# Two gate loads merged, the second gate group's sums moved into the prelude, and constants built between the first tiles, in an attention and mixture-of-experts kernel

## The chip, the cores and the metric

One core of one Trainium2 chip. The metric is the device time of one launch in microseconds; for the kernel before, three runs gave a median of 797.4 us (796.29 to 798.65).

## The reference

Three parts follow one another. The first is a gated recurrence over 768 steps for 4 batches of 8 heads of 40 values; the kernel computes it in chunks of 128 steps.

```python
def _attn_ref(q, k, v, i_gate, f_gate, o_gate):
    ...
    for t in range(S):
        m_new = np.maximum(f_gate[:, :, t] + m, i_gate[:, :, t])
        f_stab = np.exp(f_gate[:, :, t] + m - m_new)
        i_stab = np.exp(i_gate[:, :, t] - m_new)
        m = m_new
        C = f_stab[:, :, None, None] * C + i_stab[:, :, None, None] * np.einsum('bhd,bhe->bhde', vt, kt)
        n = f_stab[:, :, None] * n + i_stab[:, :, None] * kt
        h_tilde = np.einsum('bhde,bhe->bhd', C, qt)
        nq = np.einsum('bhd,bhd->bh', n, qt)[:, :, None]
        denom = np.maximum(np.abs(nq), 1.0)
        o = 1.0 / (1.0 + np.exp(-o_gate[:, :, t]))
        y[:, :, t] = o * h_tilde / denom
```

Its 3072 rows of 320 go to a router with 8 experts of capacity 384 each (assignment in falling order of all logits), through the expert's two layers with a rectifier between them, and then through a second pair of layers, 320 to 2048 to 320, with a leaky rectifier. The output is 3072 x 320.

## The kernel before

The program is written by hand for each engine; the order on an engine is the order of its block in the code, and engines meet by semaphores alone. SyncE (SP) issues nearly all loads. Tiles are counted by chunk `c` (6 of them, 128 steps each) and batch `b` (4): tile (c, b) is T = 4c + b, 24 in all.

**Gates.** The running sums of the forget gate, the running maximum and what follows from them are computed ahead for many chunks at once, with (chunk, batch, head) on the partitions: group 0 holds chunks 0 to 3 (128 partitions), group 1 chunks 4 and 5 (64 partitions). `load_gates` (L408) and L959 load them, one DMA per chunk and gate. On VectorE (DVE), `gate_sums(g)` (L1127) makes the sums, `split_peak(g)` (L1142) three bf16 parts of the peak, `fade_weights(g)` (L1154) a diagonal of carry weights, `copy_gates(g)` (L1159) and `copy_fades` (L1167) bring the turned results out of PSUM. ScalarE (ACT) makes exponentials (`gate_weights`, L961) and places the peak parts (`place_peak`, L968). TensorE (PE) turns them (`turn_gates`, L642) and spreads the fade weights over the heads (`spread_fades`, L650).

**A tile.** On PE, `front` (L664) makes the logarithms of the decays (L675) and the scores k.q (L684) of the next tile; `back` (L699) the product with the carried state (L713, from chunk 1 on), the update of the state (L720), the router's logits of the tile two before (L695) and probabilities times v (L732); `turn_x` (L736) turns the output of the tile before (L742). ACT takes exponentials of the decays (L992). DVE multiplies decays and scores (`make_probs`, L1248), then normalises and gates the output of the tile before (`make_x`, L1264), whose first steps read PSUM and write the state. GpSimd (POOL) weighs v (`vw`, L557), masks the probabilities (L563) and fades the state (L570), in `weigh_values` (L548). The loop is software-pipelined by one tile: `step` (L745 on PE, L1306 on DVE, L1010 on ACT) makes the next tile's front before this tile's back. The first four steps are written out; group 1's gate work is hung into them: before the change the sums follow the output of tile (0,0), the split that of (0,1), the fade weights that of (0,2), and the copies that of (0,3); PE turns group 1 in the step of tile (0,3).

**Constants.** POOL fills `ident`, `sel3`, the zero padding and `half_ones`, then all the constants of the routing and of its search (L513 to L546), and only then starts on the tiles (L592).

After tile 23 come the routing search and eight experts, each expert's matmuls in three passes over high and low parts.

## Time and profile before

| what | value |
|---|---|
| median of 3 runs | 797.4 us (796.29 to 798.65) |
| the profiled execution | 797.02 us |
| its span in the trace | 795.3 us |
| PE busy | 741.7 us, 93% of the span |
| DVE busy | 583.1 us, 73% |
| ACT busy | 323.0 us, 41% |
| POOL busy | 160.7 us, 20% |

The span reaches from the first to the last instruction of the trace; 1.7 us of the execution lie outside it. Busy shares are means over stages: attention takes the first 156 us of the span, the routing search and the first rows of an expert some 45 us, the experts the rest.

### The profile page before, as it was taken

The numbers are of one execution on the slowest core, as the hardware profiler recorded it, in microseconds if no ns is written. First come the engines' busy times: TensorE is split into PE (matmuls) and PEld (weight loads), VectorE is DVE, ScalarE is ACT, GpSimd is POOL, SyncE is SP. The second block draws the span as 40 slices with busy tenths as digits, with TensorE's granted clock in tenths as the row PEclk, the third lists the DMA queues.
The fourth block names the chain that finished last, engine by engine and source line by source line (L and its number), as shares of the span: only waits on it lengthen the run. The fifth ranks groups of instructions, "written<-read, shape, count | busy, mean of one in ns | idle before, by whom it ended". The sixth has DMA issues, their size and how long they took to land.

```text
span 795.3 us, 18189 instructions
## 1 busy us (share of the span) xinstructions
PE 741.7 (93%) x6047; PEld 692.6 (87%) x6047; DVE 583.1 (73%) x1615; ACT 323.0 (41%) x775; POOL 160.7 (20%) x240
## 2 busy tenths in 40 slices
PE   5899999752899999999999999999999999999995
PEld 4799999742789998998999899989988998999994
DVE  5878888858578867886887688678867876883442
ACT  5666777301324513441452236134414532361431
POOL 7367777101000220110022002200110220021001
PEclk9999999955899999999999999999999999999998
DMA  6889886103204100400140041004000500310000
GB/s 148 225 251 241 228 228 167 37 12 109 67 2 147 31 26 1 156 26 19 46 129 25 0 132 43 25 0 146 29 25 22 153 25 0 122 52 26 1 1 25
DMA packets 66706, 62.54 MB, mean 79 GB/s; under 512 B 34928, under 2 KB 57840, under 8 KB 66672
## 3 DMA queue, kind: packets, MB, share of 16 engines
q1 hardware_dynamic: 56880, 48.66, 21.6%
q0 software_dynamic: 2688, 8.65, 3.4%
q10 hardware_dynamic: 7104, 4.79, 1.9%
q8 instruction: 20, 0.33, 0.2%
q14 instruction: 14, 0.11, 0.1%
HBM read 53.43 MB, written 8.65 MB: 78 GB/s over the span
## 4 chain that ended last, share of the span: by engine, by line
PE 85%; DVE 8%; issue 2%; ACT 2%; DMA 1%; ACTq 1%; POOL 0%; DVEq 0%; POOLq 0%
PE bank L844 21%; PE bank L846 18%; PE bank L845 18%; PE bank L862 4%; PE bank L863 4%; PE bank L732 4%; PE bank L695 2%; PE bank L713 2%; PE bank L684 2%; PE bank L887 1%; PE bank L888 1%; PE bank L767 1%; PE bank L776 1%; PE bank L838 1%; ACT decay L992 1%
## 5 line engine op out<-in xcount | busy, mean ns | idle before, releaser
L844 PE MATMUL bank<-wo_hi,h_hi 128*128 128x320 f32 x384 | 120.7, 314 | 0.0
L846 PE MATMUL bank<-wo_hi,h_lo 128*128 128x320 f32 x384 | 118.6, 309 | 0.0
L845 PE MATMUL bank<-wo_lo,h_hi 128*128 128x320 f32 x384 | 118.0, 307 | 0.0
L611 POOL DMA_INDIRECT xe<-x_rows,idx_in x24 | 31.1, 1294 | 402.3 <-DVE idx_in L1442 353.4
L1502 DVE SCALAR_TENSOR_TENSOR g_act<-g_neg,rest_alpha,bank 128x384 f32<-128x384 f32 x128 | 78.6, 614 | 39.3 <-ACT g_neg L1075 37.7
L1075 ACT ACTIVATE g_neg<-bank 128x384 f32<-128x384 f32 x128 | 62.8, 491 | 102.1 <-PE bank L863 102.1
L1073 ACT ACTIVATE h_hi<-bank 128x384 fp32r<-128x384 f32 x64 | 31.5, 492 | 163.4 <-PE bank L863 163.4
L1079 ACT CAST h_hi<-g_act 128x384 fp32r<-128x384 f32 x128 | 65.5, 512 | 78.8 <-DVE g_act L1502 78.3
L844 PE MATMUL bank<-yT_hi,wi_hi 128*128 128x384 f32 x256 | 92.4, 361 | 0.3 <-DVE yT_lo L1528 0.3
L845 PE MATMUL bank<-yT_lo,wi_hi 128*128 128x384 f32 x256 | 86.8, 339 | 0.0
L846 PE MATMUL bank<-yT_hi,wi_lo 128*128 128x384 f32 x256 | 86.7, 339 | 0.0
L1507 DVE TENSOR_TENSOR h_lo<-g_act,h_hi 128x384 fp32r<-128x384 f32 x128 | 71.1, 555 | 17.0 <-ACT h_hi L1079 13.3
L844 PEld LDWEIGHTS bank<-wo_hi,h_hi 128*128 128x128 f32 x384 | 72.3, 188 | 0.0
L845 PEld LDWEIGHTS bank<-wo_lo,h_hi 128*128 128x128 f32 x384 | 72.2, 188 | 0.0
L846 PEld LDWEIGHTS bank<-wo_hi,h_lo 128*128 128x128 f32 x384 | 72.0, 188 | 0.0
L622 POOL DMA_INDIRECT out<-out_sb,idx_out x24 | 30.1, 1255 | 173.4 <-DVE out_sb L1575 168.5
L1497 DVE SCALAR_TENSOR_TENSOR h_lo<-bank,h_hi 128x384 fp32r<-128x384 f32 x64 | 35.3, 552 | 25.1 <-ACT h_hi L1073 25.1
L992 ACT ACTIVATE decay<-bank,aT 128x128 f32<-128x128 f32 x192 | 52.2, 383 | 3.7 <-PE bank L675 1.6
L844 PEld LDWEIGHTS bank<-yT_hi,wi_hi 128*128 128x128 f32 x256 | 48.1, 188 | 3.9 <-DVE yT_lo L1528 2.0
L844 PE MATMUL bank<-xT_hi,w_hi 128*128 128x384 f32 x128 | 50.7, 396 | 0.8 <-DVE xT_lo L1489 0.8
L844 PE MATMUL bank<-h_hi,w_hi 128*128 128x384 f32 x128 | 48.0, 375 | 1.1 <-DVE h_lo L1497 1.1
L845 PEld LDWEIGHTS bank<-yT_lo,wi_hi 128*128 128x128 f32 x256 | 48.2, 188 | 0.0
(227 smaller groups left out, 1743.0 us busy)
## 6 DMA issues: line engine op xcount, KB each, us to landing
s<-w SPq DMA_DIRECT2D x8, 1280.0 KB, 9.1
s<-w SPq DMA_DIRECT2D x8, 1024.0 KB, 5.3
s<-w SPq DMA_DIRECT2D x16, 256.0 KB, 6.0
k_in<-kT SPq DMA_DIRECT2D x48, 80.0 KB
q_in<-qT SPq DMA_DIRECT2D x48, 80.0 KB
k_row<-k SPq DMA_DIRECT2D x24, 160.0 KB, 3.4
v_in<-v SPq DMA_DIRECT2D x24, 160.0 KB, 3.8
gate_o<-o SPq DMA_DIRECT2D x24, 160.0 KB, 3.2
```

What stands on the lines that cost most here:

```text
L732: ins = pe.matmul(YB[:, at:at + WIDE], probs[:, n, half, y, :], v_in[:, b, :, :].rearrange("p h d -> p (h d)")[:, D1 * h:D1 * h + WIDE], s ...
L844: pe.matmul(acc, ah, bh, start=start, stop=False, skip_group_check=True)
L845: pe.matmul(acc, ah, bl, start=False, stop=False, skip_group_check=True)
L846: return pe.matmul(acc, al, bh, start=False, stop=stop, skip_group_check=True)
L862: pe.matmul(acc, wh[:, 2, js], ah[:, 2, :], start=False, stop=False, skip_group_check=True)
L863: pe.matmul(acc, rest[:, js], al[:, 2, :], start=False, stop=True, skip_group_check=True).then_inc(up_ready, 1)
L992: ins = act.activation(decay[:, half, y, :], LOGD[half][:, P * y:P * y + P], ACT.Exp, bias=aT[:, c, h:h + 1])
L1075: act.activation(g_neg[:, :], acc, ACT.Relu, scale=-1.0).then_inc(act_ready, 1)
L1079: act.copy(h_hi[:, k % 3, :], g_act[:, k % 3, :]).then_inc(g_hi, 1)
L1497: dve.scalar_tensor_tensor(out=h_lo[:, n, :], in0=acc, scalar=0.0, in1=h_hi[:, n, :].bitcast(F32), op0=ALU.max, op1=ALU.subtract).then_inc ...
L1502: dve.scalar_tensor_tensor(out=g_act[:, n, :], in0=g_neg[:, :], scalar=rest_alpha[:, j:j + 1], in1=acc, op0=ALU.mult, op1=ALU.add).then_in ...
L1507: dve.tensor_tensor(h_lo[:, n, :], g_act[:, n, :], h_hi[:, n, :].bitcast(F32), ALU.subtract).then_inc(h_ready, 1)
```

## The change

Four edits, all at the head of the program:

1. Each gate group comes with one DMA per gate instead of one per chunk.
2. DVE runs `gate_sums(1)` in the prelude, right after `copy_gates(0)`; the split, the fade weights, the turning and the copies of group 1 move one step sooner each, and on DVE they stand between `make_probs` of the next tile and `make_x` of this one instead of behind `make_x`. ACT's `gate_weights(1)` moves from step 1 to step 0, PE's `turn_gates(1)` and `spread_fades` from the step of tile (0,3) to that of (0,2).
3. PE makes the update of tile (0,0) between the decay logarithms and the scores of tile (0,1).
4. POOL builds the constants of routing and search in three pieces, behind its work on tiles (0,0), (0,1) and (0,2).

```diff
-                for c in GROUPS[group]:
-                    eng.dma_start(dst[bh_rows(c), group, :], src.rearrange("b h s -> (b h) s")[:, P * c:P * c + P]).then_inc(gates_in[group], 16)
+                cs = GROUPS[group]
+                eng.dma_start(dst[0:HB * len(cs), group, :],
+                              src.rearrange("b h (c p) -> c (b h) p", p=P)[cs.start:cs.stop]).then_inc(gates_in[group], 16)
...
             pool.sem_inc(prep_lo, 4)
-            for b in range(B):
-                weigh_values(0, b)
+            weigh_values(0, 0)
+            routing_consts()
+            weigh_values(0, 1)
+            search_consts()
+            weigh_values(0, 2)
+            mask_consts()
+            weigh_values(0, 3)
...
+            def update(c, b):
+
+                T = B * c + b
+                n = b % 2
+                if first(T, 1):
+                    pe.wait_ge(consts, 4)
+                pe.wait_ge(kv_in[b], 32 * (c + 1))
+                if not final(T):
+                    pe.wait_ge(vw_ready, T + 1)
+                for y in range(HP if not final(T) else 0):
+                    for u in range(2):
+                        pe.matmul(UPDATE[ROWS * u:ROWS * u + D, D1 * y:D1 * y + D1], k_row[:, b, D * (HP * u + y):D * (HP * u + y) + D],
+                                  vw[:, n, head(u, y), :], start=True, stop=True)
...
-                if first(T, B) and b == 3:
+                if first(T, B) and b == 2:
                     turn_gates(1)
                     spread_fades()
...
-                if not isinstance(T, int) or T + 1 < NT:
+                if first(T, 1):
+                    logds(c, b + 1)
+                    update(c, b)
+                    scores(c, b + 1)
+                elif not isinstance(T, int) or T + 1 < NT:
                     front(*nxt(c, b))
...
-            for c in GROUPS[0]:
-                act.dma_start(gate_i[bh_rows(c), 0, :], i_gate.rearrange("b h s -> (b h) s")[:, P * c:P * c + P]).then_inc(gates_in[0], 16)
+            act.dma_start(gate_i[:, 0, :], i_gate.rearrange("b h (c p) -> c (b h) p", p=P)[0:4]).then_inc(gates_in[0], 16)
...
-                    if b == 1:
+                    if b == 0:
                         gate_weights(1)
...
-            dve.wait_ge(gates_in[0], 128)
+            dve.wait_ge(gates_in[0], 32)
             gate_sums(0)
             split_peak(0)
             copy_gates(0)
+            dve.wait_ge(gates_in[1], 32)
+            gate_sums(1)
...
                     make_probs(*nxt(c, b))
+                if first(T, B):
+                    if b == 0:
+                        split_peak(1)
+                    if b == 1:
+                        fade_weights(0)
+                        fade_weights(1)
+                    if b == 2:
+                        dve.wait_ge(gates_turned, 3)
+                        copy_gates(1)
+                        copy_fades()
                 if not isinstance(T, int) or T < NT:
                     make_x(c, b)
-                if first(T, B):
-                    if b == 0:
-                        dve.wait_ge(gates_in[1], 64)
-                        gate_sums(1)
-                    if b == 1:
-                        split_peak(1)
-                    if b == 2:
-                        fade_weights(0)
-                        fade_weights(1)
-                    if b == 3:
-                        copy_gates(1)
-                        copy_fades()
```

`routing_consts`, `search_consts` and `mask_consts` hold the instructions of L513 to L546, unchanged and in the same order.

On DVE, from the copies of gate group 0 on, this stands before the change:

```order
L1164 COPY gT<-bank 128x128
L1254 TENSOR_TENSOR probs<-decay,bank 128x512 [waits scores_ready,decay_ready] x4
L1275 COPY hsum<-bank 128x2x4x41 [waits y_done]
L1289 COPY state<-bank 128x164
L1295 SCALAR_TENSOR_TENSOR nq<-hsum 128x8 [waits out_read]
L1296 TENSOR_SCALAR norm<-nq 128x8 [waits dve_step]
L1297 RECIPROCAL rnorm<-norm 128x8 [waits dve_step]
L1298 TENSOR_TENSOR scaled<-hsum,rnorm 128x320 [waits dve_step]
L1302 SCALAR_TENSOR_TENSOR x_sb<-gate_o,scaled 128x320 [waits tanh_ready,dve_step]
L1130 SCALAR_TENSOR_TENSOR cum_f<-ones_row,gate_f 64x128 [waits gates_in1]
```

and this with it:

```order
L1195 COPY gT<-bank 128x128
L1161 SCALAR_TENSOR_TENSOR cum_f<-ones_row,gate_f 64x128 [waits gates_in1]
L1162 TENSOR_TENSOR log_in<-gate_i,cum_f 64x128 [waits gate_step]
L1163 SCALAR_TENSOR_TENSOR peak<-log_in 64x128 [waits gate_step]
L1168 SCALAR_TENSOR_TENSOR carry<-peak,carry,cum_f 32x1 [waits gate_step] x2
L1170 SCALAR_TENSOR_TENSOR neg_peak<-peak,carry,minus_row 64x128 [waits gate_step]
L1287 TENSOR_TENSOR probs<-decay,bank 128x512 [waits scores_ready,decay_ready] x4
L1178 CAST peak_parts<-neg_peak 64x128 [waits gate_logs]
L1180 TENSOR_TENSOR neg_a<-neg_peak,peak_parts 64x128 [waits parts_ready]
L1181 CAST peak_parts<-neg_a 64x128 [waits gate_step]
L1183 TENSOR_TENSOR peak_parts<-neg_a,peak_parts 64x128 [waits parts_ready]
L1308 COPY hsum<-bank 128x2x4x41 [waits y_done]
```

The five rows of group 1's sums now stand ahead of the first probabilities, and its split ahead of the first output (`hsum`).

On PE, around the first tile's update (`k_row`, L720), before:

```order
L675 MATMUL bank<-peak_111,sel_112 128x128 [waits decay_ready]
L675 MATMUL bank<-peak_111,sel_112 128x128 x3
L684 MATMUL bank<-q_in,k_in 128x128 [waits qk_in1,probs_ready]
L684 MATMUL bank<-q_in,k_in 128x128 x7
L720 MATMUL bank<-vw,k_row 40x41 [waits vw_ready,kv_in0,consts]
L720 MATMUL bank<-vw,k_row 40x41 x7
L732 MATMUL bank<-v_in,probs 128x128 [waits masked]
```

with the change:

```order
L687 MATMUL bank<-peak_111,sel_112 128x128 [waits decay_ready]
L687 MATMUL bank<-peak_111,sel_112 128x128 x3
L731 MATMUL bank<-vw,k_row 40x41 [waits vw_ready,kv_in0,consts]
L731 MATMUL bank<-vw,k_row 40x41 x7
L700 MATMUL bank<-q_in,k_in 128x128 [waits qk_in1,probs_ready]
L700 MATMUL bank<-q_in,k_in 128x128 x7
L760 MATMUL bank<-v_in,probs 128x128 [waits masked]
```

The update is now issued ahead of the scores (`q_in,k_in`) of tile (0,1), which wait for the first probabilities.

On PE in the step of tile (0,2), with the change (before, the rows from `ident,log_in` to `half_ones` stood in the step of tile (0,3), at the same place of it):

```order
L716 MATMUL bank<-wg_sb,xT_sb 128x96 [waits xT_copied,consts_in]
L716 MATMUL bank<-wg_sb,xT_sb 128x96 x2
L659 MATMUL bank<-ident,log_in 128x64 [waits gate_exps]
L660 MATMUL bank<-ident,g_row 128x64
L661 MATMUL bank<-ident,w_row 128x64
L670 MATMUL bank<-fade_diag,half_ones 128x64 [waits diag_ready,consts]
L670 MATMUL bank<-fade_diag,half_ones 128x64
L670 MATMUL bank<-fade_diag,half_ones 128x32 x2
L760 MATMUL bank<-v_in,probs 128x128 [waits masked]
```

Turning and spreading of group 1 now stand between the router's rows and the probabilities times v of tile (0,2).

## Rows read from the trace of the kernel before

**Rows 1.** The page: span, and the clock granted to PE in 40 slices.

```profile
span 795.3 us, 18189 instructions
...
PEclk9999999955899999999999999999999999999998
```

**Rows 2.** Windows: length, busy us (count) by engine, granted clock, DMA share, GB/s.

```profile
20.00:30.00 10.00, 8.67 (x120) 7.96 (x119) 9.48 (x28) 7.49 (x27) 3.85 (x6) 1.00 0.89 248
...
37.60:60.00 22.40, 22.34 (x299) 21.12 (x300) 15.96 (x38) 13.73 (x48) 14.55 (x23) 1.00 0.91 249
```

**Rows 3.** Timeline, PE: start, us, instructions, [idle before, releaser].

```profile
13.34 1.18 PE L684 MATMUL bank<-q_in,k_in 64*128 64x128 f32 x16 [0.49 <-DVE probs L1254]
14.44 0.51 PE L720 MATMUL bank<-vw,k_row 128*40 128x41 f32 x16
...
23.07 1.16 PE L684 MATMUL bank<-q_in,k_in 64*128 64x128 f32 x16 [1.32 <-DVE probs L1254]
...
31.36 1.19 PE L657 MATMUL bank<-fade_diag,half_ones 128*128 128x64 f32 x8 [0.50 <-DVE fade_diag L1157]
...
37.66 1.16 PE L713 MATMUL bank<-state,q_in 64*128 64x123 f32 x16 [1.26 <-DVE fade L1170]
```

**Rows 4.** Timeline, DVE: zero fills, gate sums, probabilities, fade weights.

```profile
1.52 0.48 DVE L1116 MEMSET q_in<- 128x512 f32 x1
...
4.58 0.43 DVE L1130 TENSOR_TENSOR_SCAN cum_f<-ones_row,gate_f 128x128 f32<-128x128 f32 x1 [1.16 <-DMA gate_i<-i_gate]
...
12.00 1.28 DVE L1254 TENSOR_TENSOR probs<-decay,bank 128x512 f32<-128x512 f32 x2 [2.61 <-PE bank L684]
...
16.97 0.50 DVE L1275 COPY hsum<-bank 128x328 f32<-128x328 f32 x1 [1.05 <-PE bank L732]
...
19.19 0.99 DVE L1130 TENSOR_TENSOR_SCAN cum_f<-ones_row,gate_f 64x128 f32<-64x128 f32 x1
...
21.75 1.27 DVE L1254 TENSOR_TENSOR probs<-decay,bank 128x512 f32<-128x512 f32 x2
...
25.75 0.21 DVE L1147 CAST peak_parts<-neg_peak 64x128 bf16<-64x128 f32 x1
...
26.78 1.27 DVE L1254 TENSOR_TENSOR probs<-decay,bank 128x512 f32<-128x512 f32 x2
...
30.78 0.43 DVE L1157 TENSOR_SCALAR fade_diag<-ident,g_row 128x128 f32<-128x128 f32 x2
```

**Rows 5.** Timeline, POOL: constants, and vw of tiles (0,0) and (0,2).

```profile
7.13 0.20 POOL L513 MEMSET ones_bf<- 128x128 bf16 x1
...
8.65 0.10 POOL L529 MEMSET flag<- 128x1 bf16 x1
...
9.94 0.11 POOL L538 MEMSET tmp_a<- 128x31 f32 x1
...
12.11 0.73 POOL L557 TENSOR_TENSOR vw<-v_in,wT 128x328 f32<-128x328 f32 x1
...
19.17 0.73 POOL L557 TENSOR_TENSOR vw<-v_in,wT 128x328 f32<-128x328 f32 x1 [2.45 <-DMA v_in<-v]
```

**Rows 6.** Timeline, SP's queue: DMA issues.

```profile
2.65 0.72 SPq L425 DMA_DIRECT2D k_in<-kT  x2
...
5.99 0.90 SPq L411 DMA_DIRECT2D gate_i<-i_gate  x2
...
18.55 0.35 SPq L428 DMA_DIRECT2D k_row<-k  x1
```

**Rows 7.** Landings: k_row of tile (0,3); all v_in up to 50 us.

```profile
DMA to landing us min/median/max: 3.2/3.2/3.2
...
DMA to landing us min/median/max: 3.1/3.6/5.1
```

**Rows 8.** Packets, 8.75 to 11.15 us (four 40-row loads); q1, whole span.

```profile
DMA packets 297, 0.45 MB, mean 186 GB/s; under 512 B 45, under 2 KB 137, under 8 KB 297
...
q1 hardware_dynamic: 56880, 48.66, 21.6%
```

More of the change, by code:

```diff
@@ L530, in _ @@
-            ch.mark(pool.memset(above, 0.0))
-            ch.link(pool.memset(step_size[:, :], 0.0))
-            for n, (bits, shift) in enumerate(STEPS):
-                J = 2 ** bits - 1
-                pool.memset(step_size[0:J, n:n + 1], float(2 ** shift))
-            pool.iota(steps[:, 0, :], pattern=[[1, JM]], base=1, channel_multiplier=0,
-                      allow_small_or_imprecise_dtypes=True).then_inc(consts, 1)
-            ch.mark(pool.memset(same_step, 0.0))
-            ch.link(pool.memset(own_block[:, :, :], 1.0))
@@ L540, in _ @@
-            for n in range(4):
-                ch.link(pool.affine_select(out=same_step, in_=same_step, compare_op=ALU.not_equal, fill=1.0,
-                                           base=-n * JM, pattern=[[-1, JM]], channel_multiplier=1))
-            ch.link(pool.affine_select(out=own_block[:, :, :], in_=own_block[:, :, :], compare_op=ALU.is_ge, fill=0.0, base=0,
-                                       pattern=[[-JM, 4], [0, E]], channel_multiplier=1))
-            pool.affine_select(out=own_block[:, :, :], in_=own_block[:, :, :], compare_op=ALU.is_ge, fill=0.0, base=JM - 1,
-                               pattern=[[JM, 4], [0, E]], channel_multiplier=-1).then_inc(consts, 1)
@@ new lines, in search_consts @@
+            def search_consts():
+                ch.mark(pool.memset(flag[:, :], 0.0))
+                ch.mark(pool.memset(above, 0.0))
+                ch.link(pool.memset(step_size[:, :], 0.0))
+                for n, (bits, shift) in enumerate(STEPS):
+                    J = 2 ** bits - 1
+                    pool.memset(step_size[0:J, n:n + 1], float(2 ** shift))
+                pool.iota(steps[:, 0, :], pattern=[[1, JM]], base=1, channel_multiplier=0,
+                          allow_small_or_imprecise_dtypes=True).then_inc(consts, 1)
@@ new lines, in mask_consts @@
+            def mask_consts():
+                ch.mark(pool.memset(same_step, 0.0))
+                ch.link(pool.memset(own_block[:, :, :], 1.0))
+                for n in range(4):
+                    ch.link(pool.affine_select(out=same_step, in_=same_step, compare_op=ALU.not_equal, fill=1.0,
+                                               base=-n * JM, pattern=[[-1, JM]], channel_multiplier=1))
+                ch.link(pool.affine_select(out=own_block[:, :, :], in_=own_block[:, :, :], compare_op=ALU.is_ge, fill=0.0, base=0,
+                                           pattern=[[-JM, 4], [0, E]], channel_multiplier=1))
+                pool.affine_select(out=own_block[:, :, :], in_=own_block[:, :, :], compare_op=ALU.is_ge, fill=0.0, base=JM - 1,
+                                   pattern=[[JM, 4], [0, E]], channel_multiplier=-1).then_inc(consts, 1)
@@ L662, in _, with logds @@
             turn_gates(0)
-            def front(c, b):
+            def logds(c, b):
                 T = B * c + b
-                n = b % 2
                 if b == 0:
@@ L677, in front, with scores @@
                     ins.then_inc(logd_ready, 1)
+            def scores(c, b):
+                T = B * c + b
                 if not first(T, 1):
@@ L686, in front @@
                 ins.then_inc(scores_ready, 1)
+            def front(c, b):
+                logds(c, b)
+                scores(c, b)
             def prev(c, b, k):
@@ L714, in back @@
                                   state[half_rows(u), HP * b + y:HP * b + y + 3, :].rearrange("p y d -> p (y d)"), start=True, stop=True)
-                pe.wait_ge(kv_in[b], 32 * (c + 1))
-                if not final(T):
-                    pe.wait_ge(vw_ready, T + 1)
-                for y in range(HP if not final(T) else 0):
-                    for u in range(2):
-                        pe.matmul(UPDATE[ROWS * u:ROWS * u + D, D1 * y:D1 * y + D1], k_row[:, b, D * (HP * u + y):D * (HP * u + y) + D],
-                                  vw[:, n, head(u, y), :], start=True, stop=True)
+                if not first(T, 1):
+                    update(c, b)
                 if not first(T, 2):
```

32 lines of the change are left out of this document (16 added, 16 removed).

## The prediction

> **What bounds the kernel now.** Read the page first: span 795.3 us, and PE's granted clock, full in all slices but three in the routing search and the last [rows 1], which the change leaves alone. Then the windows of the attention stage: from 37.6 to 60 us PE is busy 22.34 of 22.40 us, from 20 to 30 us only 8.67 of 10, while DVE is busy 9.48 of 10 [rows 2]. So from tile (1,0) on PE sets the pace, and everything behind follows it; before that DVE does. The changed work lies wholly in front of 37.66 us, where PE first multiplies with the carried state [rows 3], so the question is by how much that moment moves. The timelines of PE and DVE say what holds it. PE sits idle 0.49 us before the scores of tile (0,1), 1.32 before those of (0,3), 0.50 before it spreads the fade weights and 1.26 before the carried product, each time released by DVE [rows 3]. On DVE stand, between the output of tile (0,0) and the next probabilities, the sums of group 1, from 19.19 to 21.75; the split from 25.75 to 26.78; and the fade weights at 30.78 [rows 4]. In the prelude the same engine was idle: 1.16 us waiting for the gate loads and 2.61 us for the first scores [rows 4].
>
> **The sum.** Take the scores of tile (0,3), at 23.07, as the first mark. (a) *Merged loads of group 0.* DVE has finished its fills at 4.58 - 1.16 = 3.42 [rows 4], so the sums can start 1.16 us sooner at most. No row has one load of 128 short rows. The nearest is v_in, 128 partitions in one load: median 3.6 us from issue to landing, longest 5.1 [rows 7]. Issued at about 0.8, that is 4.4, with 5.9 as the bad end. The load is smaller (64 KB against 160), so I take 0.3 us sooner, bounds 1.16 sooner and 1.3 later. (b) *Sums of group 1 in the prelude.* 21.75 - 19.19 = 2.56 us [rows 4], of which the first scan's 0.99, against 0.43 for group 0, coincides with POOL's vw at 19.17 [rows 5]. They go into the 2.61 us before the first probabilities. Their loads are now issued after one SP wait: k_in of tile (0,0) may go when the zero fill of 1.52 + 0.48 = 2.00 is done [rows 4] instead of at 2.65, and two issues of 0.45 us are saved at 5.99 [rows 6], so SP runs 0.65, then 1.55 us ahead. Group 1 is then issued at about 5.3 and 5.8; with 3.6 us it is there at 9.4, when DVE is through with the copies of group 0. The gap is thus filled exactly: net 0, bounds +0.3 (loads earlier) and -1.5 (landing as slow as 5.1). (c) *Update of (0,0) first.* It goes into the 0.49 us gap before the scores of (0,1); the scores start at 13.34 and the update, 14.44 to 14.88, no longer lies between them and the probabilities times v: 0.44 us [rows 3]. (d) *DVE's sums gone from before the probabilities of (0,2).* DVE could start them 2.56 us sooner, but PE gains only its idle time, 1.32 us; next due is PE's own row of work. DVE itself comes close: the split, 1.03 us, now precedes the output of (0,0), where DVE was idle 1.05 us at 16.97 [rows 4], and with (c) only 0.61 of that is left. The probabilities of (0,2) thus come 2.56 + 0.3 + 0.44 - (1.03 - 0.61) = 2.9 us sooner; 0.3 + 0.44 + 1.32 = 2.1 are wanted. Scores of (0,3): 23.07 - 0.3 - 0.44 - 1.32 = 21.0.
>
> (e) *Loads of tile (0,3)* must be there by then. Its k_row, behind q_in in the queue, was issued at 18.55 and landed 3.2 us later, at 21.75 [rows 6, 7]. DMA's mean share is 0.89 from 20 us on [rows 2], so this is a queue that is full, not only issued. If it moves with SP's 1.55 us it lands at 20.2, if it does not move at all, at 21.75 and the gain shrinks by 0.75. I take it as moved.
>
> (f) *From the scores of (0,3) to the carried product*, 23.07 to 37.66, PE waited 0.50 + 1.26 = 1.76 us [rows 3]. With the fade weights made a step sooner on DVE and copied ahead of the output of (0,2), both waits have nothing left to wait for; PE's work between the marks is the same, only in another order: 21.0 + 14.59 - 1.76 = 33.8. What is late next: the turning and spreading, some 1.2 us and more, now delay the product of (0,2), not that of (0,3); DVE waits for them at `gates_turned` with the output of (0,2) queued behind, but that output needs the product, which PE issues after the turning anyway. Probabilities of (0,3), queued before that wait, are needed only at the scores of (1,0), more than 2 us later.
>
> (g) *POOL's constants.* 12.11 - 7.13 = 4.98 us: 1.52 routing, 1.29 search, 2.17 mask [rows 5]. Removed from before vw of (0,0), they give nothing, since PE did not wait for POOL. Placed between tiles they lie in waits of POOL for probabilities and for v_in (2.45 us at 19.17). Cover gone, vw of the next tile would be late by the piece, at most 2.17 us; the mask piece comes after tile (0,2), and vw of (0,3) is not wanted until the update of (0,3), some 6 us later. Cost 0. (h) ACT's two exponentials and the order of the peak copies: 0, in its waits for PE.
>
> Sum: 0.3 + 0.44 + 1.32 + 1.76 = 3.8 us. Behind 37.66 PE is the pace, so all of it should arrive at the end. The profiled execution took 797.02 us, which makes 793.2; the median of the runs is 0.4 us higher, so I forecast **793.6 us**. A difference below 0.3%, 2.4 us, can hardly be told from none.
>
> **A rule that speaks against the merged loads.** Four 40-row loads lie in the window from 8.75 to 11.15 us, with at most 45 packets under 512 B [rows 8]: if each load wrote a completion packet on all 16 engines there would be 64. The Trainium skill (DMA: Bandwidth & Descriptors, Why a DMA increments its semaphore by 16 and not by 1) says that a load runs on the largest number of engines up to 16 that divides the slowest dimension of both sides. By it a 40-row load uses 10 engines, 40 completion packets for four, with which the trace agrees; and the merged loads, whose source has the chunk outermost, would use 4 engines for group 0 and 2 for group 1.
>
> **Rivals.** *K, the gate loads on few engines.* The merged loads' rows may sit on few engines and hold up what is queued behind. One packet of q1 took 0.216 x 16 x 795.3 / 56880 = 48 ns of an engine in the mean [rows 8]. If the 128 rows of group 1's two loads lie on two engines, that is 64 x 48 ns = 3.1 us there, and tile loads behind them need all engines. If none of it is caught up, k_row and q_in of (0,3) land at 20.2 + 3.1 = 23.3, 2.3 us after 21.0: gain 1.5, 795.9 us. For it: DMA is 0.89 busy. Against it: the issues of tile 1 and 2 leave room to catch up. This is what the rule just cited would do here. *L, the loads of (0,3) stay where they are*, being bound by the DMA engines: gain 3.8 - 0.75 = 3.05, or 2.4 if q_in lands after k_row: 794.7 us. *C, POOL's constants hold DVE.* A scan took 0.99 instead of 0.43 us beside vw [rows 4, 5]. Were DVE stopped in that way for the whole of the first two pieces, 2.81 us, less the 0.8 of slack left in (d), gain 1.8, 795.6 us. Against it: the constants mostly write only, and in the prelude they ran beside DVE without a like loss. The Trainium skill (SBUF — State Buffer, Who interferes with whom) has only POOL instructions that read SBUF block a DVE instruction with two SBUF inputs; by it the first piece would cost at most its one selection. *S, slower.* As K, and the queue behind also slows from the shortest landing of v_in to its longest, 5.1 - 3.1 = 2.0 us [rows 7]: 3.1 + 2.0, less the 0.8 that the loads have in hand, puts the scores of (0,3) at 25.3, that is 4.3 - 3.8 = 0.5 us slower, 797.9 us; it decides from the point where q_in of (0,3) lands after 24.8. *N, the change does less than it says*: group 1's gates land so late (past 11 us) that DVE's new wait merely replaces the old sums; gain about 2, counted with K.
>
> **Chances.** Forecast 0.57, its own range 792.4 to 794.9; L 0.12; K with N 0.16; C 0.11; S 0.04. Faster by over 0.3%: forecast, most of L and a little of K, 0.73; within 0.3%: 0.23; slower by over 0.3%: 0.04. The range takes in L, K and C and leaves the worst of K and C and all of S out: 792.2 to 796.2.
>
> **What the profile would show.** Right: the sums of group 0 start before 4.5 and those of group 1 right behind the copies of `gT`, ending before 12; nothing but the probabilities follows the output of (0,0) on DVE; scores of (0,3) at 20.5 to 21.5; no idle time of PE before it spreads the fades; the carried product at 33.3 to 34.3; steps of about 6 us as before from there. Wrong: a DMA wait on DVE before group 1's sums longer than 1 us, a wait of PE for q_in at (0,3) (K, L, S), DVE's scans or casts stretched beside POOL (C), or a later stage that is longer by what the first one lost.

## The result, and the profile after

The kernel with the change takes 795.4 us (median of 12 runs, 794.5 to 797.4), the kernel before, on the same chip, 797.1 us (12 runs, 796.2 to 800.0): ratio 0.9976, 95% interval 0.9965 to 0.9988. It is faster, by 1.7 us and not by the 3.8 us forecast; 795.4 lies in the range of 792.2 to 796.2, and the gain is under the 0.3% that the prediction called hard to tell from none. The profiled executions differ by 1.3 us of span, 794.0 against 795.3.

The page after reads like the one before [rows 1]: the same three slices at a lower granted clock in the routing search.

```profile
span 794.0 us, 18182 instructions
...
PEclk9999999955899999999999999999999999999998
```

So the question is one of three or four us within the first 60. The stretch up to the first carried product, at tile (1,0), is called the front below. Timeline of PE after, first tiles (start, us, instructions, [idle before, releaser]):

```profile
13.67 1.16 PE L700 MATMUL bank<-q_in,k_in 64*128 64x128 f32 x16 [0.96 <-DVE probs L1287]
14.76 2.05 PE L760 MATMUL bank<-v_in,probs 128*128 128x128 f32 x16
...
18.97 0.51 PE L731 MATMUL bank<-vw,k_row 128*40 128x41 f32 x16 [0.61 <-DVE hsum L1308]
...
22.16 1.16 PE L700 MATMUL bank<-q_in,k_in 64*128 64x128 f32 x16
23.89 0.51 PE L731 MATMUL bank<-vw,k_row 128*40 128x41 f32 x16 [0.57 <-DVE hsum L1308]
...
25.50 1.22 PE L670 MATMUL bank<-fade_diag,half_ones 128*128 128x64 f32 x8
...
35.35 1.06 PE L746 MATMUL bank<-state,q_in 64*128 64x123 f32 x16
```

The four waits of before [rows 3] have changed: the one ahead of the scores of (0,1) is 0.96 us and starts them 0.33 later, those of 1.32, 0.50 and 1.26 are gone, and two new ones, 0.61 and 0.57 us, stand ahead of the updates of (0,1) and (0,2), both for `hsum`. The first carried product begins at 35.35 for 37.66 [rows 3], 2.31 us sooner.

DVE after, answering to [rows 4]:

```profile
4.81 0.42 DVE L1161 TENSOR_TENSOR_SCAN cum_f<-ones_row,gate_f 128x128 f32<-128x128 f32 x1 [1.39 <-DMA gate_i<-i_gate]
...
9.91 0.87 DVE L1161 TENSOR_TENSOR_SCAN cum_f<-ones_row,gate_f 64x128 f32<-64x128 f32 x1 [0.30 <-DMA gate_f<-f_gate]
...
12.35 1.27 DVE L1287 TENSOR_TENSOR probs<-decay,bank 128x512 f32<-128x512 f32 x2
...
16.15 0.53 DVE L1178 CAST peak_parts<-neg_peak 64x128 bf16<-64x128 f32 x1
16.72 0.61 DVE L1180 TENSOR_TENSOR neg_a<-neg_peak,peak_parts 64x128 f32<-64x128 f32 x1
...
18.15 0.48 DVE L1308 COPY hsum<-bank 128x328 f32<-128x328 f32 x1
...
20.67 1.28 DVE L1287 TENSOR_TENSOR probs<-decay,bank 128x512 f32<-128x512 f32 x2
21.86 1.42 DVE L1188 TENSOR_SCALAR fade_diag<-ident,g_row 128x128 f32<-128x128 f32 x2
23.08 0.48 DVE L1308 COPY hsum<-bank 128x328 f32<-128x328 f32 x1
```

The sums of group 0 begin later (4.81 for 4.58), those of group 1 fit into the old gap, and the split (16.15 to 18.15) and the fade weights now stand ahead of `hsum` and last 2.00 and 1.42 us instead of 1.03 and 0.43.

The rest goes later. The product of each tile with v_in (L732 before, L760 after) is a good ruler; its starts are 5.95 us apart in most tiles: before it begins at 45.97, 52.07 and 58.01 for the sixth to eighth tile, after at 43.57, 49.52 and 57.12. The lead of 2.55 us shrinks to 0.89 in one step of 7.60 us. ACT's instructions and DMA issues (ACTq) at that place:

```profile
46.05 0.36 ACTq L1038 DMA_DIRECT2D x_rows<-x_sb  x1
46.18 0.26 ACT L1036 COPY xT_sb<-bank 64x128 f32<-64x128 f32 x1
46.57 2.11 ACTq L1039 DMA_DIRECT2D x_rows<-x_sb  x1
48.73 0.47 ACT L1030 ACTIVATE gate_o<-gate_o 128x320 f32<-128x320 f32 x1 [2.30 <-issue]
```

One issue of an x store, 0.35 us in most tiles, took 2.11, and `gate_o`, the casts and the next decays stood behind it; PE then waits for a decay and for probabilities:

```profile
52.72 0.40 PE L687 MATMUL bank<-peak,sel 128*128 x4 [0.56 <-ACT decay L1023]
53.52 1.16 PE L700 MATMUL bank<-q_in,k_in 64*128 64x128 f32 x16 [0.40 <-DVE probs L1287]
```

In the view of the DMA queues for 46.6 to 48.3 us (queue, kind: packets, MB, share of the 16 engines) stands one packet of a queue that is seldom there. It is 16 KB of instructions, begins at 46.62 and takes 1.67 us:

```profile
q8 instruction: 1, 0.02, 6.1%
```

From there the lead stays at 0.88 us to the last v_in product (151.29 for 152.17). At the end of the span it is 1.3.

### The profile page after: what moved, and what is told of

It is laid out like the page before. It is cut to its first block, busy times and chain, and to the rows that moved or that the text cites. A ratio compares the mean times of both kernels' runs of the same rounds, so it can differ in the third digit from the quotient of the medians.

```text
span 794.0 us, 18182 instructions
## 1 busy us (share of the span) xinstructions
PE 740.8 (93%) x6047; PEld 692.1 (87%) x6047; DVE 583.3 (73%) x1615; ACT 322.5 (41%) x775; POOL 160.8 (20%) x240
## 3 DMA queue, kind: packets, MB, share of 16 engines
q1 hardware_dynamic: 56760, 48.66, 21.5%
## 4 chain that ended last, share of the span: by engine, by line
PE 84%; DVE 7%; issue 3%; ACT 2%; DMA 2%; ACTq 1%; SPq 0%; POOL 0%; DVEq 0%; POOLq 0%
PE bank L876 21%; PE bank L878 18%; PE bank L877 18%; PE bank L894 4%; PE bank L895 4%; PE bank L760 3%; PE bank L716 2%; PE bank L746 2%; PE bank L700 2%; PE bank L919 1%; PE bank L920 1%; PE bank L799 1%; PE bank L808 1%; ACT decay L1023 1%; PE bank L870 1%
## 5 line engine op out<-in xcount | busy, mean ns | idle before, releaser
L878 PEld LDWEIGHTS bank<-yT_hi,wi_lo 128*128 128x128 f32 x256 | 48.1, 188 | 0.0
```

Source lines behind the costliest of these rows:

```text
L878: return pe.matmul(acc, al, bh, start=False, stop=stop, skip_group_check=True)
```

## The experiments

Twelve kernels ran, four at a time, each four on another chip and beside the kernel before (medians 796.5, 796.4 and 796.8 us). For each the table has its median and ratio to the kernel before with its interval, and from its trace: the start of group 0's first sum, of the first, fifth ((1,0)), eighth and 24th v_in product, and the span, in us.

| kernel | median | ratio (95%) | cum_f | 1st | 5th | 8th | 24th | span |
|---|---|---|---|---|---|---|---|---|
| before | 797.1 | | 4.58 | 14.88 | 39.92 | 58.01 | 152.17 | 795.3 |
| the change | 795.4 | 0.9976 (0.9965-0.9988) | 4.81 | 14.76 | 37.52 | 57.12 | 151.29 | 794.0 |
| the change again | 795.27 | 0.9981 (0.9971-0.9990) | 5.31 | 14.94 | 37.69 | 56.69 | 150.82 | 793.5 |
| loads per chunk | 794.75 | 0.9974 (0.9964-0.9984) | 4.19 | 14.14 | 37.40 | 56.27 | 150.48 | 793.7 |
| constants in front | 794.20 | 0.9969 (0.9956-0.9982) | 5.25 | 15.16 | 37.36 | 55.89 | 150.05 | 792.6 |
| update first alone | 797.37 | 1.0011 (0.9996-1.0025) | 4.30 | 14.52 | 39.39 | 57.33 | 151.46 | 793.8 |
| sums alone | 796.31 | 0.9985 (0.9973-0.9997) | 4.20 | 14.31 | 39.02 | 56.97 | 151.16 | 793.7 |
| split late | 794.71 | 0.9971 (0.9960-0.9981) | 5.06 | 14.90 | 37.01 | 55.45 | 149.62 | 793.0 |
| turned late | 794.58 | 0.9972 (0.9961-0.9983) | 4.99 | 14.50 | 36.62 | 55.98 | 150.15 | 793.0 |
| x rows by SP | 799.20 | 1.0023 (1.0010-1.0037) | 4.90 | 14.95 | 37.60 | 55.54 | 153.28 | 795.6 |
| three with SP | 798.90 | 1.0026 (1.0013-1.0040) | 4.99 | 15.18 | 36.60 | 55.37 | 154.08 | 796.9 |
| stores ahead | 792.97 | 0.9942 (0.9925-0.9959) | 5.20 | 14.84 | 37.59 | 55.53 | 148.43 | 791.4 |
| combined | 792.02 | 0.9930 (0.9914-0.9947) | 5.63 | 15.30 | 36.81 | 54.76 | 147.64 | 790.5 |
| combined, chunk loads | 793.46 | 0.9951 (0.9933-0.9970) | 4.30 | 16.40 | 38.39 | 56.34 | 149.21 | 792.1 |

How to read it: the first columns vary from execution to execution (4.81 and 5.31, 14.76 and 14.94 for the changed kernel), so parts of the start are best compared between columns (from the first product to the fifth). The stretch behind the 24th product is 642.3 to 643.4 us in all fourteen: nothing of this study acts there.

**The change again.** No edit.

> The changed kernel once more, as it is. In its first trace the carried product of (1,0) began 2.31 us sooner than before (35.35 for 37.66), the probs of tile (1,3)'s time, 52.07 before, 2.55 us sooner, and then 1.66 us of it were gone at 57.12 (58.01 before): ACT's issue of the 32 KB x_rows part took 2.11 us at 46.57 where it takes 0.35. Theory A (that issue waits for an instruction packet: one of 16 KB began at 46.62 and took 1.67 us): a fixed place of the program, so the issue is long again, within 1 us of 46.6, and the sixth product with v_in begins some 0.9 us sooner than before; the ratio is 0.9976 again. Theory B (an accident of that one run, by the load of the DMA engines): no issue above 0.7 us there, the lead at that product is 2.4 to 2.6 us, and the profiled span is 1.7 us shorter, some 792.4.

Neither theory as written. No long issue at 46.6, but one of 1.54 us at 40.71, and again an instruction packet lies there: 16 KB, from 40.62 to 41.88. SP's own issue at the same time is as long:

```profile
40.71 1.54 ACTq L1039 DMA_DIRECT2D x_rows<-x_sb  x1
40.72 1.62 SPq L433 DMA_DIRECT2D gate_o<-o  x1
```

The step from the sixth to the seventh product took 7.01 us, so 1.06 us was lost. The place moves, the pairing with a packet does not.

**Loads per chunk.** The change, with twelve loads of 32 rows for the four merged ones.

```diff
-                cs = GROUPS[group]
-                eng.dma_start(dst[0:HB * len(cs), group, :],
-                              src.rearrange("b h (c p) -> c (b h) p", p=P)[cs.start:cs.stop]).then_inc(gates_in[group], 16)
+                for c in GROUPS[group]:
+                    eng.dma_start(dst[bh_rows(c), group, :], src.rearrange("b h s -> (b h) s")[:, P * c:P * c + P]).then_inc(gates_in[group], 16)
```

> The changed kernel with its gate loads as before, one per chunk (twelve issues for four). Theory A (the merged load costs: cum_f of group 0 began 0.23 us later than before, and group 1's neg_peak let the probs of (0,0) begin at 12.35 for 12.00): cum_f of group 0 begins at 4.6 again, the first probs at 12.0 to 12.1, the carried product of (1,0) 0.2 to 0.4 us sooner than 35.35, the time 0.2 to 0.4 us below the changed kernel's. Rival (twelve issues hold SP and the second group longer: its loads took 3.94 us from issue to landing merged, and 1.79 us of SP's issuing for 1.09): group 1's sums wait for the loads, the probs of (0,0) come after 12.35, and the time is the same or up to 0.5 us longer.

Theory A as to the start: first sum at 4.19. Over all traces the merged load gives 4.81 to 5.63 (nine, mean 5.1), the chunks 4.19 to 4.58 (five, mean 4.3): merging *costs* 0.8 us there. But the 0.62 us won at the first product (14.14 for 14.76) are 0.12 at the fifth (37.40 for 37.52), for now PE waits for `q_in`:

```profile
17.57 1.16 PE L699 MATMUL bank<-q_in,k_in 64*128 64x128 f32 x16 [0.92 <-DMA q_in<-qT]
...
22.69 1.16 PE L699 MATMUL bank<-q_in,k_in 64*128 64x128 f32 x16 [0.77 <-DMA q_in<-qT]
```

All three kernels with twelve gate issues and a quicker front have these two waits (0.74 to 0.92 us), at the same moments, 17.5 to 17.8 and 22.7 to 22.9; none with the merged loads has them. SP issues k_in of (0,3) at 15.71 in the changed kernel and at 16.58 here. What merging gives is SP's time, and what it takes is the landing of the gates. Of the time as a whole, 0.5 us below the changed kernel, the intervals overlap.

**Constants in front.** The change, with `routing_consts`, `search_consts` and `mask_consts` called ahead of `weigh_values(0, 0)`.

```diff
-            weigh_values(0, 0)
             routing_consts()
-            weigh_values(0, 1)
             search_consts()
-            weigh_values(0, 2)
             mask_consts()
+            weigh_values(0, 0)
+            weigh_values(0, 1)
+            weigh_values(0, 2)
             weigh_values(0, 3)
```

> The changed kernel with POOL's constants built ahead of its first tile, as before, and all else changed. Theory C (POOL's constants between the tiles stretch what DVE does beside them: the split of group 1 took 2.00 us for 1.03, fade_diag 1.42 for 0.43, and TensorE waited 0.61 and 0.57 us for hsum): both go back to about 1.0 and 0.5 us, one of the two waits goes, and the time is 0.5 to 1.1 us below the changed kernel's. Rival (they are stretched by POOL's weighing and masking of the tiles, which stand beside them anyway): split and fade_diag stay above 1.6 and 1.0 us, and the time is the changed kernel's within 0.3 us, or longer by what POOL's weighing of tile (0,0) comes later.

Theory C in part, and the rival as to the split. The split still takes 2.09 us, the fade weights 0.92 for 1.42; of the two waits for `hsum` the second goes, the first is 0.71. From first to fifth product it is 22.20 us for 22.76, so 0.56 sooner. What stands beside the split in both kernels is POOL's weighing and masking of the tiles, which the change did not move: it moved the split beside them. Beside the fade weights too it is mainly masking (21.89 to 23.11 in the changed kernel, 21.70 to 22.92 here), only differently placed, so that the constants themselves took the 0.50 us is not shown. The small copies of 64x128 are 0.21 us when POOL is idle and 0.53 beside it, the subtraction from 0.28 to 0.61. (The Trainium skill, SBUF — State Buffer, Who interferes with whom, has a VectorE instruction with two SBUF inputs, and copies and casts in their two-port modes, contend with GpSimd for a shared port; with that the subtraction's 0.61 us beside a reading POOL agrees.) The rest of the 1.1 us in the medians is not in the front: see the eighth product, and the DMA issues below.

**Update first, alone.** The kernel before, the update of (0,0) ahead of the scores of (0,1).

```diff
-                if not isinstance(T, int) or T + 1 < NT:
+                if first(T, 1):
+                    logds(c, b + 1)
+                    update(c, b)
+                    scores(c, b + 1)
+                elif not isinstance(T, int) or T + 1 < NT:
                     front(*nxt(c, b))
```

> The kernel before with one part of the change alone: the update of tile (0,0) runs ahead of the scores of (0,1). All theories: it fills 0.44 us of TensorE's wait of 0.49 us for the probs at 13.34, so all that follows comes 0.4 us sooner; the carried product of (1,0) at 37.2 to 37.3 for 37.66. If TensorE is the pace behind it the time is 0.4 us below the kernel before's; if the lead at 37 us is partly lost at 40 to 60 us, as the changed kernel's was (1.66 of 2.55 us), 0.1 to 0.2 us.

The fifth product comes 0.53 us sooner, of which 0.28 is the earlier first sum. PE waits for `q_in` here as well (0.74 and 0.76 us), which takes what the update gave. In time there is no gain: the interval holds 1. Its twelve runs scatter from 795.3 to 799.9 us, as those of the kernel before do, and the traced one, 795.5 us, is among the quickest: the span in the table is not its typical one.

**Sums alone.** The kernel before with `gate_sums(1)` in the prelude.

```diff
             copy_gates(0)
+            dve.wait_ge(gates_in[1], 64)
+            gate_sums(1)
...
-                    if b == 0:
-                        dve.wait_ge(gates_in[1], 64)
-                        gate_sums(1)
```

> The kernel before with one part of the change alone: group 1's sums in the prelude (2.56 us of VectorE's work, in its idle 2.61 us ahead of the first probs). Prediction's step (d): TensorE's wait of 1.32 us for the probs at 23.07 goes, the waits of 0.50 and 1.26 us for fade_diag and fade stay, and the time is 1.0 to 1.3 us below the kernel before's. Rival (with twelve gate issues the loads of tiles (0,2) and (0,3) are next: TensorE waited 0.74 to 0.92 us for q_in at 17.6 and at 22.8 in two traces of such kernels): the wait at 23.07 becomes one of 0.5 to 0.9 us for q_in, and the gain is 0.2 to 0.7 us.

The rival. The wait of 1.32 us for probabilities [rows 3] is gone and has become these; the wait for `fade` (1.26) stays:

```profile
17.55 1.16 PE L684 MATMUL bank<-q_in,k_in 64*128 64x128 f32 x16 [0.74 <-DMA q_in<-qT]
...
22.78 1.16 PE L684 MATMUL bank<-q_in,k_in 64*128 64x128 f32 x16 [0.87 <-DMA q_in<-qT]
```

From the first product to the fifth it gives 0.33 us (24.71 for 25.04), not 1.32. The sums pay only together with SP's saved issues.

**Split late.** The change, with `split_peak(1)` behind `make_x` of tile (0,2).

```diff
-                    if b == 0:
-                        split_peak(1)
                     if b == 1:
...
                     make_x(c, b)
+                if first(T, B) and b == 2:
+                    split_peak(1)
```

> The changed kernel with group 1's peak split into its three parts behind tile (0,2)'s x instead of ahead of tile (0,0)'s. Theory D (VectorE's work ahead of hsum is what TensorE waits for: 0.61 us at 18.97 and 0.57 us at 23.89, each for hsum; the split took 2.0 us there and stands now where VectorE was idle 2.2 to 2.9 us): the first wait goes whole and the second whole or in part, scores of (0,3) begin at 21.5 to 21.8 for 22.2 to 22.3, the carried product of (1,0) 0.6 to 1.2 us sooner, the time 0.6 to 1.2 us below the changed kernel's (795.3). Rival (TensorE itself or the loads are next): the waits move to q_in or to the masks, and the time changes by under 0.3 us.

Theory D in half: the wait at 18.97 is gone, that at 23.89 is still 0.62 us, behind a fade_diag of 1.42. From first to fifth product 22.11 us, 0.65 sooner. The same four instructions take 1.03 us at their new place. In time 0.6 us below the changed kernel, intervals overlapping.

**Turned late.** The change, with group 1 turned and spread at (0,3), and VectorE's fade weights and copies a tile later, still ahead of `make_x`.

```diff
-                if first(T, B) and b == 2:
+                if first(T, B) and b == 3:
                     turn_gates(1)
...
-                    if b == 1:
+                    if b == 2:
                         fade_weights(0)
...
-                    if b == 2:
+                    if b == 3:
                         dve.wait_ge(gates_turned, 3)
```

> The changed kernel with group 1 turned, faded and copied a tile later again, at tile (0,3), and all else changed. Prediction's step (f) (turning a tile sooner takes away TensorE's waits of 0.50 and 1.26 us for fade_diag and fade): both come back, about 0.3 to 0.5 and 1.2 us, while the new wait of 0.57 us for the hsum of (0,1) goes since fade_diag no longer stands ahead of it; the carried product of (1,0) 1.0 to 1.4 us later and the time 0.8 to 1.4 us above the changed kernel's. Rival (the later stretch takes the gain back, as 1.66 us was lost at 46 to 58): the product is later but the time only 0 to 0.5 us above.

Both wrong, and the most useful run for step (f). No wait for `fade_diag` or `fade` comes back; the wait at the update of (0,2) is gone, and the fifth product is 22.12 us behind the first, not 22.76:

```profile
23.00 0.51 PE L731 MATMUL bank<-vw,k_row 128*40 128x41 f32 x16
...
29.55 1.22 PE L670 MATMUL bank<-fade_diag,half_ones 128*128 128x64 f32 x8
...
34.45 1.06 PE L746 MATMUL bank<-state,q_in 64*128 64x123 f32 x16
```

So the 1.76 us of (f) came from VectorE's pieces standing ahead of `make_x` instead of behind it (the only part of (f) that this run keeps). Turning a tile sooner added nothing, and cost 0.57 us at the update. And again, later:

```profile
45.67 1.87 ACTq L1039 DMA_DIRECT2D x_rows<-x_sb  x1
```

with an instruction packet from 45.63 to 47.16.

**x rows by SP.** The change, with both stores of a tile issued by SP, behind its wait for x.

```diff
                     sp.wait_ge(x_ready, T - B + 1)
+                    store_x(c - 1, b)
                 sp.dma_start(gate_o[:, b, :], o[T]).then_inc(o_in[b], 16)
...
+            for b in range(B):
+                sp.wait_ge(x_ready, NT - B + b + 1)
+                store_x(NCH - 1, b)
```

`store_x` holds ACT's two issues.

> The changed kernel with the two x_rows stores of a tile issued by SP, behind its wait for x, instead of by ACT. Theory I (an issue that meets a 16 KB instruction packet ends only 0.4 us after it: 48.68 for 48.29, 42.25 for 41.87, 47.84 for 47.43 in three traces; on ACT such an issue of 1.0 to 2.1 us holds the decays, and 0.6 to 1.7 us of the lead goes between the third and fourth tile of the loop's first round): SP's issues meet the packets, ACT's don't exist, the loss at 43 to 58 us is under 0.3 us, and the time is 0.6 to 1.6 us below the changed kernel's; ACT's 0.7 us of issuing per tile may give 0.5 us more. Rival (the loss there is by transfers or by SP, or SP's seven issues a tile become the pace): the fourth-to-seventh v_in products keep a step above 6.5 us, and the time is the same or longer by 0.5 to 2 us.

Both at once. The eighth product comes at 55.54, the steps before it are 5.94 to 6.05 us: the loss at 43 to 58 us is gone. From 60 us on SP, now with two issues more a tile, is the pace:

```profile
71.78 1.16 PE L710 MATMUL bank<-q_in,k_in 64*128 64x128 f32 x16 [1.45 <-DMA q_in<-qT]
```

Five such waits, of 0.58 to 1.45 us, to the end of the stage.

**Three with SP.** Constants in front, split late, stores by SP.

> The changed kernel with three of the edits together: POOL's constants ahead of its tiles, the split of group 1 behind tile (0,2)'s x, and x_rows stored by SP. If each acts by itself: 1.1 us (constants, measured 794.2 for 795.3) and 0.6 to 1.2 us and 0.6 to 1.6 us below the changed kernel, 791.8 to 793.0. If the first two fill the same two waits (0.61 and 0.57 us for hsum), they give 1.2 us together and the time is 792.5 to 793.6.

A miss, for the reason just given, with eight waits for `q_in` (0.34 to 2.08 us). From first to fifth product it is 21.42 us, so the first two edits do add up (1.3 us).

**Stores ahead.** ACT's two issues ahead of its wait for the turned x, where it has no work.

```diff
+                act.wait_ge(x_ready, T + 1)
+                act.dma_start(x_rows_by_tile[c, b][:, 0:DM], x_sb[:, b % 2, :]).then_inc(x_out[b % 2], 16)
+                act.dma_start(x_rows_by_tile[c, b][:, DM:3 * P], x_sb[:, b % 2, 2 * P:DM]).then_inc(x_out[b % 2], 16)
                 act.wait_ge(x_turned, T + 1)
...
-                act.dma_start(x_rows_by_tile[c, b][:, 0:DM], x_sb[:, b % 2, :]).then_inc(x_out[b % 2], 16)
-                act.dma_start(x_rows_by_tile[c, b][:, DM:3 * P], x_sb[:, b % 2, 2 * P:DM]).then_inc(x_out[b % 2], 16)
```

> The changed kernel with ACT's two x_rows stores of a tile issued ahead of its wait for the turned x, instead of behind the copies of it. Theory I (an issue that meets a 16 KB instruction packet is long; it costs where it stands ahead of the decays without slack): stores now fall into ACT's idle time (1.0 to 2.0 us ahead of the copies), so a long one of up to 2 us is absorbed; the step of TensorE that took 6.9 to 7.6 us between 49 and 57 us takes 5.95 to 6.3, and the time is 0.6 to 1.3 us below the changed kernel's (795.3). Rival (the loss there comes from transfers, and went in the run with SP's stores since these came later): a long step stays and the time is the changed kernel's within 0.3 us.

Theory I's time, and more. The eighth product is at 55.53, the time 792.97 us, 2.3 below the changed kernel. ACT's idle time now takes the issues in:

```profile
43.76 0.35 ACTq L1035 DMA_DIRECT2D x_rows<-x_sb  x1
43.87 0.41 ACT L1023 ACTIVATE decay<-bank,aT 128x128 f32<-128x128 f32 x1
44.27 0.34 ACTq L1036 DMA_DIRECT2D x_rows<-x_sb  x1
45.98 0.37 ACT L1038 COPY xT_sb<-bank 128x256 f32<-128x256 f32 x1 [1.70 <-PE bank L770]
46.25 0.26 ACT L1039 COPY xT_sb<-bank 64x128 f32<-64x128 f32 x1
46.41 0.47 ACT L1030 ACTIVATE gate_o<-gate_o 128x320 f32<-128x320 f32 x1
```

`gate_o` follows the copies at once, and of the 2.39 us by which its 24th product precedes that of the change run again, 1.16 are there at the eighth. The other 1.23 come behind it, where no long issue is: a tile in each round of the loop took 6.26 us (62.62 to 68.88) and takes 6.03 (61.46 to 67.49). With the stores on SP that tile takes 6.03 us too. So in it ACT was within a quarter of a us of the pace all along. This trace doesn't show a long issue taken in where the changed kernel lost its time: between 38 and 50 us none of ACT's is over 0.35 us. The two kernels with the same edit below do, later: issues of 0.98 us at 55.51 (combined) and 1.24 us at 57.10 (with chunk loads) leave the step of PE over them at 5.93 and 5.92 us. The six runs lie within 0.6 us (792.6 to 793.2), those of the kernels before and changed within 2.1 to 5.2, in more runs each.

**Combined.** Constants in front, split late, turned late, stores ahead.

> The changed kernel with four edits: POOL's constants ahead of its tiles, the split of group 1 behind tile (0,2)'s x, group 1 turned a tile later again, x_rows stores ahead of ACT's wait for the turned x. If both waits for hsum (0.61 and 0.57 us) go and the long step at 49 to 57 us too (0.6 to 1.6 us): the v_in product of (1,0) at 36.0 to 36.6 for 37.5 to 37.7, and the time 791.8 to 793.3. If the waits only move (to the fades or to q_in): 793.5 to 794.5.

As expected in time, 792.02 us, though its fifth product is at 36.81: its first sum was the latest of all (5.63), and the stretch between the two products, 21.51 us, has no wait of PE over 0.2 us left. Its runs (791.8 to 792.3) lie below all of stores ahead. It beats both kernels of the study, the one before by 4.8 us.

**Combined, chunk loads.** The same, group 0's gates one load per chunk, the router's weights loaded behind tile (0,2).

```diff
-                if b == 1:
+                if b == 2:
                     sp.dma_start(wg_sb[:, 0:2, :], w_gate[0:2 * P, :].rearrange("(t p) e -> p t e", p=P),
```

> The four edits of the run before it, and the loads of gate group 0 one per chunk again, with the router's weights loaded a tile later. Theory (merging group 0's loads makes its sums begin later: 4.81 to 5.31 us in seven traces with it, 4.19 to 4.58 in three without): cum_f of group 0 at 4.2 to 4.6, the first v_in product 0.4 to 0.7 us sooner than in the run before it; with the router's weights out of the way the loads of (0,2) don't become the wait, and the time is 0.3 to 0.7 us below that run's. Rival (SP's 1.05 us more of issuing delays q_in of (0,2) and (0,3)): a wait of 0.3 to 0.9 us for q_in at 17 or 22 us takes it back, the same time within 0.3 us.

A third outcome. The first sum begins at 4.30 and no `q_in` is waited for, but PE is now too early for POOL, whose constants stand in front:

```profile
13.15 0.51 PE L735 MATMUL bank<-vw,k_row 128*40 128x41 f32 x16 [1.37 <-POOL vw L527]
14.39 2.08 PE L704 MATMUL bank<-q_in,k_in 64*128 64x128 f32 x16 [0.74 <-DVE probs L1292]
```

Two waits, and then the same scores take 2.08 us for 1.16. The windows (length, busy us of PE, PEld, DVE, ACT, POOL, granted clock, DMA share, GB/s):

```profile
10.00:15.00 5.00, 2.89 (x44) 2.42 (x42) 3.67 (x8) 2.84 (x12) 3.37 (x11) 0.92 0.86 228
15.00:20.00 5.00, 5.00 (x48) 4.66 (x48) 2.19 (x6) 3.64 (x13) 2.81 (x5) 0.74 0.79 149
```

PE was busy for 2.89 of 5 us, and the granted clock fell: 0.74 in the mean of the next 5 us, so part of them at 1.2 GHz instead of 2.4. In combined PE was busy for all of the first 5 us, and the clock is 1.00 in both. With gates this early the constants should do better between the tiles, where the change has them; that version was not run.

## Why the prediction was right and wrong

**The number.** 795.4 us lies in the range of 792.2 to 796.2, but not in the forecast's own of 792.4 to 794.9; the gain is 1.7 us of 3.8. The range holds it because it took in rivals L, C and K at 794.7, 795.6 and 795.9 us, and none of them acted as written: that it held is luck as far as the mechanism goes. Of the signs that were named, PE has indeed no wait ahead of the fades and none for `q_in`, but the scores of (0,3) begin at 22.16 for 20.5 to 21.5, the carried product at 35.35 for 33.3 to 34.3, DVE's casts are stretched beside POOL, and one step takes 7.60 us for 6. About 1.5 us of the 3.8 was missing in the front, (a) to (f), and another 1.4 went behind it.

**The bound.** Right in front: DVE's order sets when PE can run, and the four waits named were the right ones. Wrong in one sentence: "Behind 37.66 PE is the pace, so all of it should arrive at the end." 2.31 us had been won there and 0.88 arrived at the last product. PE was indeed busy 22.34 of 22.40 us [rows 2], but that says nothing of the slack of the engine behind it. Stores ahead shows the slack to be nil in one tile of each round.

**(a)** 0.3 us sooner was 0.23 later in the first trace and 0.8 later over fourteen, inside the bound of 1.3 later. v_in's landings were a fair neighbour; I took the size of the load as a reason to go below them, and size was not what counted. The issue alone took 0.75 us on SP and 1.17 on ACT for 0.45 of a chunk's. Whether the rows sat on four engines, as the rule cited there would have it, can be told by the prediction's own count of completion packets. Up to 7 us ACT's queue carries `gate_i` of group 0 alone, before and after:

```profile
q10 hardware_dynamic: 192, 0.07, 3.5%
q10 hardware_dynamic: 132, 0.07, 3.1%
```

Before, that is 128 rows and 16 completion packets for each of four loads; after, 128 rows and 4. With four engines the trace agrees. The 128 packets of 27 ns came in 1.16 us, three engines' worth at work at a time. Few engines are not the whole of the delay: `gate_i`'s rows were through at 3.45 us, sooner than before (3.96), but those of `gate_f`, by SP, began at 3.12 for 1.84 and were through at 4.19 for 3.91. Why they began late stays open.

**(b)** Right: the sums fit the gap (DVE waits 0.30 us for their gates), and the first probabilities begin at 12.35 for 12.00, of which 0.23 is (a)'s.

**(c)** Right in mechanism, 0.44 us, and given back at once where `q_in` is late (update first alone).

**(d)** Scores of (0,3) at 22.16, not 21.0. The 1.32 us wait went, but the split took 2.00 us for the 1.03 counted, since its new neighbour is POOL's weighing; 0.61 us of it came back as PE's wait for `hsum`. Rival C had the mechanism with the wrong culprit: constants in front leaves the split at 2.09 us. The sentence of the page given beside it was taken for VectorE instructions with two inputs alone; two of the split's four are casts, and they were stretched as well (0.53 and 0.54 us for 0.21 and 0.22).

**(e)** Right, and more important than it was made: the loads moved, k_in of (0,3) by 1.30 us, and no merged kernel waits for `q_in` in the front. Without the merged issues (d) is worth 0.33 us. The merge was priced by its landing (a), and paid through SP's queue.

**(f)** The waits of 1.76 us went, less 0.57 for the fade weights ahead of `hsum` (1.42 us for 0.43). The prediction looked for what the sooner turning would make late among PE's products, and not at what is queued behind the new piece on DVE. Turned late shows that the turning itself was worth nothing.

**(g)** 0 was right for the time up to the scores. With the constants in front the fade weights took 0.5 us less and the second wait for `hsum` went; whether the constants did it or the place of POOL's masking is open.

**What took the rest.** 2.31 us at (1,0) and 2.55 at the seventh tile became 0.89 at the eighth when a DMA issue on ACT met an instruction packet. Its place and size differ from trace to trace: in the six traces of kernels with the changed front and ACT's stores behind the copies there is each time one long issue between 40 and 47 us (0.95 to 2.11 us, and 0.5 to 1.7 us lost between the fifth and the eighth product against 17.94 us without), in the three with the front of before none above 0.63. Two edits that only move the issues, stores ahead and x rows by SP, remove the loss, which shows ACT's issues behind the copies as its cause; that a packet makes them long rests on the fourteen traces (last section). That the change brought the meeting about, because ACT's issues came sooner and the packets by another amount, is likely from the nine traces and not shown. Nor is what made single runs of the kernel before up to 4 us longer than others; that stores ahead narrows the spread to 0.6 us was seen in six runs. Stores ahead on the kernel before was not tried, so how much of its 2.3 us needs the change is open.

## What to carry to other kernels

An engine that is 99% busy is the pace only as far as the next one has slack: read the idle time ahead of the work that feeds it, tile by tile, before passing an early gain on to the end. Put the issuing of stores where an engine waits anyway, ahead of the wait, not behind the work that the wait releases; here that one edit was worth more than the whole change. When a piece is moved on VectorE, price it by POOL's work at its new place and name what is queued behind it; when loads are merged, price the landing and the issuing queue apart, since they had opposite signs.

## What the runs showed of the hardware

A DMA issue of SP or ACT that begins while a 16 KB instruction packet is under way mostly ends some 0.4 us after that packet, whichever of the two issues it. In the changed kernel: packet to 48.29, issue to 48.68 (it began 0.05 us ahead of the packet); in its second run packet to 41.88, issues to 42.25 (ACT) and 42.33 (SP); turned late, 47.16 and 47.54; stores ahead, 47.53 and 47.93 (SP). Of 52 issues between 15 and 160 us in the fourteen traces, other than loads of 40 rows, that began more than 0.3 us into such a packet, 45 ended 0.2 to 0.6 us after it. Of 81 that began within 0.3 us of the packet's start, on either side, only 27 did, the long ones on ACT above among them; issues of 40-row loads often escape too. The packets take 0.88 to 1.67 us, and five fall between 15 and 60 us in each trace; which engine's program they carry the traces don't tell. Nor does any run move the packets alone: that the packet holds the issue, and not a third thing both, is read from how close the two ends lie.
